# Where the weight sums, the rounding remainders and the token sums of a fused attention and two-MLP kernel are made: one rearrangement across five engines

## The reference

```python
x = attn_out.transpose(0, 2, 1, 3).reshape(B * S, H * D)       # 2304 x 512
x = (sigmoid(x @ w_gate) * (x @ w_val)) @ w_out1               # 512 -> 1536 -> 512
h = x @ w_in                                                   # 512 -> 2048
out = (h * clip(h + 3, 0, 6) / 6) @ w_out2                     # 2048 -> 512
```

## Time and profile before

| | us |
|---|---|
| median of 3 runs | 1125.98 (1125.51 to 1126.51) |
| the profiled execution | 1120.71 |
| its span in the profile | 1118.9 |
| PE busy | 1074.4 (96%) |
| DVE, ACT, POOL busy | 724.5, 619.2, 526.6 |

### The profile page before, as it was taken

How to read it: one execution, slowest core, us unless ns; L and a number is a source line. 1 busy time by engine, 2 the same in 40 slices (tenths; PEclk the granted TensorE clock), 3 DMA queues, 4 the chain that set the end, 5 groups by cost and what they waited for, 6 DMA issues and landing times.

```text
span 1118.9 us, 20482 instructions
## 1 busy us (share of the span) xinstructions
PE 1074.4 (96%) x6784; PEld 995.7 (89%) x6784; DVE 724.5 (65%) x1541; ACT 619.2 (55%) x1376; POOL 526.6 (47%) x521
## 2 busy tenths in 40 slices
PE   5999999999999999999998988899999999999998
PEld 3668999999999999999998987888987889889887
DVE  5986766777776777776647445665558555675553
ACT  5787676677676677667554333533334433453333
POOL 6896666667666667666545656452223000010000
PEclk8999999999999999999999989999999999999999
DMA  8554334334334334333123755465543544454421
GB/s 183 130 129 96 93 93 120 92 93 120 93 93 120 92 92 121 93 93 100 58 66 104 247 198 196 169 226 152 159 128 99 179 116 120 113 161 122 118 61 57
DMA packets 124460, 136.99 MB, mean 122 GB/s; under 512 B 10448, under 2 KB 89808, under 8 KB 123344
## 3 DMA queue, kind: packets, MB, share of 16 engines
q1 hardware_dynamic: 124368, 135.83, 43.2%
HBM read 116.40 MB, written 19.40 MB: 121 GB/s over the span
## 4 chain that ended last, share of the span: by engine, by line
PE 89%; DVE 6%; issue 2%; DMA 1%; ACT 1%; SPq 0%; POOL 0%; DVEq 0%; ACTq 0%
PE ps L726 83%; PE ps L767 4%; PE ps L781 1%; DVE raw L1612 1%; DVE XC L1506 1%; DMA stage<-w_gate 1%; DVE Cb L1608 1%; DVE prob L1419 0%; DVE G_lo L1616 0%; DMA qk_st<-qk_t 0%; DVE AS L1514 0%; DVE AS L1515 0%; DVE AS L1516 0%; DVE Y L1586 0%; DVE h_lo L1429 0%
## 5 line engine op out<-in xcount | busy, mean ns | idle before, releaser
L726 PE MATMUL ps<-x_hi,WG 128*128 128x288 f32 x1536 | 323.7, 297 | 0.8 <-DVE pt_lo L1367 0.3
L726 PEld LDWEIGHTS ps<-x_hi,WG 128*128 128x128 f32 x1536 | 251.2, 188 | 3.1 <-issue 1.2
L726 PE MATMUL ps<-x_lo,WG 128*128 128x288 f32 x768 | 226.1, 294 | 0.0
L726 PE MATMUL ps<-XC,WC 128*128 128x384 f32 x1008 | 206.2, 340 | 10.1 <-ACT Cb L1263 3.8
L726 PEld LDWEIGHTS ps<-XC,WC 128*128 128x128 f32 x1008 | 182.2, 190 | 27.9 <-issue 11.5
L1608 DVE TENSOR_TENSOR Cb<-ps,Cb 128x384 f32<-128x384 f32 x192 | 102.4, 554 | 137.7 <-PE ps L726 94.3
L726 PE MATMUL ps<-h_hi,WO 128*128 128x288 f32 x768 | 170.4, 304 | 13.9 <-DVE h_lo L1429 13.6
L617 POOL TENSOR_TENSOR WG<-stage,WG 128x512 fp32r<-128x512 f32 x96 | 127.6, 1343 | 117.0 <-ACT WG L1088 117.0
L726 PE MATMUL ps<-wo,G_hi 128*128 128x512 f32 x540 | 168.0, 392 | 0.0
L644 POOL TENSOR_SCALAR prob<-prob,rscale 128x128 f32<-128x128 f32 (+4 forms) x160 | 110.9, 711 | 77.6 <-DVE rscale L1379 77.6
L726 PEld LDWEIGHTS ps<-x_lo,WG 128*128 128x128 f32 x768 | 144.2, 188 | 0.5
(11 more groups left out here) (127 smaller groups left out, 1989.2 us busy)
## 6 DMA issues: line engine op xcount, KB each, us to landing
WC<-w_in_parts SPq DMA_DIRECT2D x154, 256.0 KB, 2.7
stage<-w_out SPq DMA_DIRECT2D x64, 256.0 KB, 3.4
qk_st<-qk_t SPq DMA_DIRECT2D x54, 288.0 KB, 4.2
w_in_parts<-WC SPq DMA_DIRECT2D x8, 1792.0 KB, 7.4
stage<-w_gate SPq DMA_DIRECT2D x48, 256.0 KB, 3.3
stage<-w_val SPq DMA_DIRECT2D x48, 256.0 KB, 3.2
qn_st<-q_n SPq DMA_DIRECT2D x16, 256.0 KB, 3.3
raw_in<-w_in SPq DMA_DIRECT2D x16, 256.0 KB, 7.8
```

The lines of the kernel that those rows point to most:

```text
L726: return pe.matmul(o, l, r, start=start, stop=stop, skip_group_check=True)
```

## The change

1. DVE makes the sums of both pairs of a lone quarter in its first half, even e in slot 1 and odd e in slot 2. ACT rounds the odd pair at the start of the second half.
2. POOL makes remainders in seven pieces of 128x256, where it had one of 128x1280 and two of 128x256; the even pair's now come ahead of two weight blocks in the first half, the odd pair's ahead of the four blocks of the second half.
3. SP writes both pairs and loads the next two in the second half: the even pair after its first block, the odd pair after its last.
4. The token sums `XS` get five buffers (two lie where `stage` was). Those of the second chunk are made in one go after the last w_out2 tile is cut, those of the third one for each step. SP loads three w_out2 tiles for each step, and POOL holds the third tile until the seven products of step 0 are done.
5. Products 2 to 6 of step 0 go to banks 0 to 4 and don't wait for a bank; the first output units then wait for all eight additions of step 0.
6. `x_high2` and `x_lower2` come one slot later around a chunk's boundary, and the last two `x_lower2` of the first chunk come behind all copies of O0 to O7.

```diff
+    XS = [sb("XS0", [P, 2, CH], F32)]
...
-    XS = [sb(f"XS{j}", [P, 2, CH], F32) for j in two]
+    XS += [sb(f"XS{k}", [P, 2, CH], F32) for k in (1, 2)]
...
+    top[0] = stage_at
+    XS += [sb(f"XS{k}", [P, 2, CH], F32) for k in (3, 4)]
...
         def prod_bank(s, i):
-            return ps[:, MLP + (PROD * s + i) % 2, 0:CH]
+            return ps[:, MLP + (PROD * s + i) % 2 if s or i < 2 else i - 2, 0:CH]
...
+            def prepared_next(e):
+                write_parts(e)
+                if e + 2 < FP:
+                    load_raw_in(e + 2)
...
                     for x, (ahead, k) in enumerate([x for slot in CUT[p] for x in slot]):
-                        if prep is not None and prep >= 1 and x == 1:
-                            write_parts(prep - 1)
-                            if prep + 1 < FP:
-                                load_raw_in(prep + 1)
+                        if prep is not None and p == 1 and x == 1:
+                            prepared_next(prep - 1)
...
+                if prep is not None and p == 1:
+                    prepared_next(prep)
...
             for s in range(n_steps):
-                for x in (2 * s + NST, 2 * s + NST + 1):
+                for x in range(3 * s + 2 if s else NST, 3 * s + 5):
...
-            def low_ws(r, p, cut):
+            def low_ws(r, p, cut, alone):
                 for i, slot in enumerate(CUT[p]):
+                    if alone and i == (0 if p else 3):
+                        prep_lo(prepared(r, p))
...
             def prep_lo(e):
                 j = e % 2
                 pool.wait_ge(p_hi, 3 * (e + 1))
-                for at, src in ((slice(0, 5), AS[j][:, :, :]), (slice(5, 6), raw_in[j][0][:, 0:2 * P].unsqueeze(1)),
-                                (slice(6, 7), raw_in[j][1][:, 2 * P:4 * P].unsqueeze(1))):
-                    pool.tensor_tensor(WC[j][:, at, 1, :], src, WC[j][:, at, 0, :].bitcast(F32), ALU.subtract).then_inc(p_lo, 1)
+                sources = [AS[j][:, k, :] for k in range(len(SUMS))] + [raw_in[j][0][:, 0:2 * P], raw_in[j][1][:, 2 * P:4 * P]]
+                for k, src in enumerate(sources):
+                    pool.tensor_tensor(WC[j][:, k, 1, :], src, WC[j][:, k, 0, :].bitcast(F32), ALU.subtract).then_inc(p_lo, 1)
...
             for x, f in enumerate(used):
+                if x == 2:
+                    pool.wait_ge(c_prod, PROD)
...
                 for k in range(len(SUMS)):
-                    m = len(SUMS) * (c - 1) + k
-                    if m >= 2:
-                        pool.wait_ge(xs_lo, PROD * ((m - 2) // len(SUMS) + 1) + SUMS[(m - 2) % len(SUMS)] + 1)
+                    if c == 1:
+                        pool.wait_ge(w_done, n + NST)
+                    else:
+                        pool.wait_ge(c_prod, PROD * (FP * (c - 1) + 2 + k))
+                        pool.wait_ge(xs_lo, PROD * c)
                     a, b, op = x_sum_of(k, c)
-                    pool.tensor_tensor(XS[m % 2][:, :, :], a, b, op).then_inc(xs_next, 1)
+                    pool.tensor_tensor(XS[k][:, :, :], a, b, op).then_inc(xs_next, 1)
...
+                if first and c == 0:
+                    pe.wait_ge(c_add, 8)
                 if first and c >= 1:
                     pe.wait_ge(o_left, CT * (c - 1) + t + 1)
...
                 alone = not (scoring or old)
+                if alone and p == 1:
+                    prep_hi(prepared(r, p))
...
-                    if alone and i == 2 - p:
+                    if alone and p == 0 and i == 2:
                         prep_hi(prepared(r, p))
...
                 for i in range(QT):
-                    if alone and i == 1 - p:
-                        e = prepared(r, p)
+                    if alone and p == 0 and i in (1, 2):
+                        e = prepared(r, i - 1)
                         prep_sums(e)
-                        first_sums({0: (0, 1), 2: (2, 3), 4: (4,)}.get(e, ()))
+                        first_sums({0: (0,), 1: (1,), 2: (2,), 3: (3,), 4: (4,)}.get(e, ()))
...
-                            for x in {0: (0, 1, 2), 2: (3,), 4: (4,), 6: (5,), 7: (6,)}.get(j, ()) if not has_next_quarter(r) else ():
+                            for x in {0: (0, 1, 2), 2: (3,), 4: (4,)}.get(j, ()) if not has_next_quarter(r) else ():
                                 x_lower2(0, x)
...
+            x_lower2(0, 5)
+            x_lower2(0, 6)
             for s in range(n_steps):
...
                 if s >= 1:
                     g_low(s - 1, 2)
                     times_relu(s - 1, 3)
+                if ends:
+                    x_lower2(c, 4)
                 added(s, 1, 0, 1, 0)
```

More of the change, by code:

```diff
@@ L77, in attention_and_mlps @@
     Y = sb("Y", [P, DT, B * S], F32)
+    stage_at = top[0]
     stage = [sb(f"stage{j}", [P, BANK], F32) for j in range(NST)]
@@ L163, in attention_and_mlps @@
     raw_in = [[sb(f"raw_in{j}{i}", [P, BANK], F32) for i in two] for j in two]
+    top[0] = stage_at
+    XS += [sb(f"XS{k}", [P, 2, CH], F32) for k in (3, 4)]
+    assert top[0] <= region
     parts = nc.dram_tensor("w_in_parts", (FP, P, PROD * 2 * 2 * P), F32, kind="Internal").ap()
@@ L355, in x_source @@
             k = SUMS.index(i)
-            return XF[:, k, :, :] if c == 0 else XS[(5 * (c - 1) + k) % 2][:, :, :]
+            return XF[:, k, :, :] if c == 0 else XS[k][:, :, :]
         def prod_bank(s, i):
-            return ps[:, MLP + (PROD * s + i) % 2, 0:CH]
+            return ps[:, MLP + (PROD * s + i) % 2 if s or i < 2 else i - 2, 0:CH]
         def out_place(c, t):
@@ L438, in load_raw_in @@
                                  by_row_tile(w_in)[:, :, f * P:(f + 1) * P]).then_inc(p_ld[e % 2], DMA)
+            def prepared_next(e):
+                write_parts(e)
+                if e + 2 < FP:
+                    load_raw_in(e + 2)
             def write_parts(e):
-                sp.wait_ge(p_lo, 3 * (e + 1))
+                sp.wait_ge(p_lo, PROD * (e + 1))
                 sp.dma_start(parts[e, :, :], WC[e % 2][:, :, :, :].rearrange("p a b c -> p (a b c)").bitcast(F32)).then_inc(p_wr[e % 2], DMA)
@@ L528, in _ @@
                 load_out2(x)
-            write_parts(FP - 1)
             def store(c, tiles):
@@ L681, in step @@
                     phi_by_z(n)
-                low_ws(r, p, cut)
-                if not (scoring or old):
-                    prep_lo(prepared(r, p))
+                low_ws(r, p, cut, not (scoring or old))
             wait_qk(0)
@@ L704, in _ @@
             for x, f in enumerate(used):
+                if x == 2:
+                    pool.wait_ge(c_prod, PROD)
                 if x == EARLY:
-                    pool.wait_ge(p_lo, 3 * FP)
+                    pool.wait_ge(p_lo, PROD * FP)
                     pool.wait_ge(xs_lo, PROD)
@@ L981, in product @@
                 if i == 0 and s < 2:
-                    pe.wait_ge(p_lo, 3 * (FP - 1 + s))
+                    pe.wait_ge(p_lo, PROD * (FP - 1 + s))
                 elif i == 0:
@@ L988, in product @@
                     pe.wait_ge(f_y, OU * (n_pairs + 1) - 1 + g)
-                else:
-                    s0, i0 = divmod(g - 2, PROD)
+                elif g >= PROD:
+                    s0, i0 = divmod(g - 2, PROD) if g >= PROD + 2 else (0, (1, 0)[g - PROD])
                     if i0 < 2:
@@ L1303, in _ @@
                     x_high2(c + 1, 0)
-                    x_high2(c + 1, 1)
                 relu(s, 1)
                 if next_x:
-                    x_high2(c + 1, 2)
+                    x_high2(c + 1, 1)
                 g_high(s, 1)
                 if next_x:
-                    x_high2(c + 1, 3)
+                    x_high2(c + 1, 2)
                 if ends:
@@ L1315, in _ @@
                 if next_x:
-                    x_high2(c + 1, 4)
+                    x_high2(c + 1, 3)
                 if ends:
@@ L1322, in _ @@
                     leave(c - 1, 4)
+                if next_x:
+                    x_high2(c + 1, 4)
                 relu(s, 3)
@@ L1511, in prep_sums @@
                 if e >= 2:
-                    dve.wait_ge(p_lo, 3 * (e - 1))
+                    dve.wait_ge(p_lo, PROD * (e - 1))
                 (a11, a12), (a21, a22) = [[t[:, k * 2 * P:(k + 1) * 2 * P] for k in two] for t in raw_in[j]]
@@ L1638, in _ @@
                     x_lower2(c + 1, 0)
-                    x_lower2(c + 1, 1)
                 times_relu(s, 1)
@@ L1644, in _ @@
                 if next_x:
-                    x_lower2(c + 1, 2)
+                    x_lower2(c + 1, 1)
                 added(s, 5, 2, 4, 5)
                 if next_x:
-                    x_lower2(c + 1, 3)
+                    x_lower2(c + 1, 2)
                 times_relu(s, 2)
@@ L1651, in _ @@
                 if next_x:
-                    x_lower2(c + 1, 4)
+                    x_lower2(c + 1, 3)
             g_low(n_steps - 1, 2)
```

## The result

The changed kernel takes 1116.09 us (median of 4 runs, 1114.99 to 1117.08) where the kernel before, run beside it, takes 1125.74 (4 runs, 1123.46 to 1126.51): a ratio of 0.9917, 95% interval 0.9899 to 0.9935, or 9.65 us gained. The forecast was 1114.8. A second timing beside other runs of before gave 1113.89, ratio 0.9911 (0.9895 to 0.9926).

What follows compares the result with a forecast made beforehand. PE was taken as the bound, with 89% of the chain. Terms 5.3 + 1.9 + 5.0 - 1.0 = 11.2 us took the profiled 1120.7 to 1109.5, or 1114.8 against the median; range 1100 to 1121.

Steps and rivals of the forecast that it cites:

- the four terms: Lone quarters 5.3 us gained, second MLP's start 1.9 gained, boundaries 5.0 gained, mid-chunk sums 1.0 lost.
- The three waits for `h_lo` go: Lone quarters: PE's three waits and their low clock vanish, 19.7 us removed.
- V0 waits for the odd sums: Second to fourth lone quarters: late odd raw tiles make PE wait 5.0, 2.1 and 2.6 us.
- the working: Lone-quarter reckoning: even write at 616.0, odd raw tiles usable 17.0 us later, 14.4 us standing in place of 19.7.
- The lone quarters gain 5.3: Lone quarters: 10.0 us of waits and 4.4 of low clock replace 19.7; bounds 16.0 to -0.1.
- The start of the second MLP gains 1.9: Second MLP's start: 14.7 us in place of 16.6, from 1 lost to 4.5 gained.
- DVE's way of 11.3 us: Second MLP's start: DVE's time to all eight additions, 2.8 + 6.5 + 2.0 us, taken as 12.1 beside POOL's cuts.
- Boundaries gain 5.0: Chunk boundaries: 0.2 of each 2.7 us idle stays, 5.0 us gained, bounds 2.7 and 5.4.
- Five sums in mid-chunk lose 1.0: Mid-chunk: five token sums of 2.15 us in a row cost PE 1.0 us, between 0 and 4.
- The rival of 4 us lost: Mid-chunk: five sums in a row block DVE, PE loses 4 us, not 1; time 1117.8, chance 0.11.
- The rival in which the odd raw tiles are hidden anyway: Lone quarters: V0 passes in time, only 0.3 of 19.7 us stays; time 1100.7, chance 0.17.
- The slower rival: Lone quarters: raw tiles later still, nothing gained from 2.3 us delay, 1134.1 at 5; chance 0.05 loss, 0.07 no change.

Runs made afterwards that it cites:

- loads first: Changed kernel, with SP asking for a pair's next raw tiles ahead of that pair's write instead of behind it: 1108.54 us.
- writes last: Changed kernel, with both writes of a lone quarter behind all its loads (raw tiles and w_out1 blocks): 1105.07 us.
- large pieces: Changed kernel, with POOL's remainders in one piece of 128x1280 and two of 128x256 as before: 1112.88 us.
- two banks: Changed kernel, with step 0 of the second MLP in two PSUM banks again, without the wait for all eight additions: 1110.48 us.
- early w_out2: Changed kernel, with SP's first three w_out2 loads ahead of the last write: 1114.18 us.
- after again: Changed kernel without an edit, timed a second time: 1113.89 us, ratio 0.9911.
- Token sums alone: Kernel before, plus only five token-sum buffers, sums in mid-chunk and the later `x_high2` and `x_lower2`: 1116.69 us, ratio 0.9930.
- the two other edits: Changed kernel with both writes behind the loads, plus step 0 in two banks and first w_out2 loads ahead of the last writes: 1102.58 us.

## Why the prediction was right, point by point

The direction and the mechanism in the lone quarters were right, and the time lay 1.3 us from the forecast. The time was partly luck: two of the four terms came out well below their size, and the medians show some 3 us that no term accounts for.

- *The three waits for `h_lo` go.* Right: none is left in after.
- *V0 waits for the odd sums, since the raw tiles stand behind the even write, three blocks and the odd write.* Right, and shown by loads first and writes last. The tiles were usable 18.7, 17.9 and 17.5 us after the even write, where the working had 17.0; the sums took 3.4 to 4.1 us, inside its 2.1 to 4.7. The even write itself came at 619.17, where the working had 616.0; 1.9 of these 3.2 us are the later beginning of the quarters, the rest POOL's way to it. The waits were 2.93, 2.32 and 3.63 us, 8.9, where it had 5.0, 2.1 and 2.6, 9.7. The first lone quarter has no gap (0.3 expected).
- *The lone quarters gain 5.3.* Too much: by the profiles it is 1.9. The step that was mis-sized is the cost of the late queue. The working let only DVE wait behind it, but ACT does too: a w_out1 block behind the even write held a gate copy for 2.39 us. PE, late by that and by the low clock behind it, waited less for V0 there: with large pieces, where the gate copy's gap was 0.35 us, V0's was 4.70, near the 5.0 of the working; with gate-copy gaps of 2.1 to 3.8 us (after, two banks, early w_out2, after again) it was 2.9 to 3.6. Idle time was 11.3 us for 10.0, and the half-speed stretches lost 1.7, 3.1 and 1.7 us, 6.5 for 4.4 (each is its length times what its clock lacks, as from 642.60: 6.20 x 0.50). So 17.8 us stand in place of 19.7, inside the bounds given (16.0 to -0.1).
- *The start of the second MLP gains 1.9.* Wrong in sign: 1.0 lost, at the edge of its bounds. The first gap is 1.1 us (0.4 expected), from the first product to the first output unit 738.90 - 725.10 = 13.8 (12.1), and 2.7 are lost to the clock behind it (2.2): 17.6 in place of 16.6. The step that failed is DVE's way of 11.3 us, for which 0.8 us more were taken beside POOL's cuts: four operations of 0.50 to 0.55 us took 0.96 to 1.45 there, and in early w_out2, with most of the cuts out of the way, the stretch was 12.4 us, near the 12.1. Two banks in step 0 gave 4 and 5 us back, so the five banks together with their wait for all eight additions cost more than they save; the two were not tried apart.
- *Boundaries gain 5.0.* Right: 5.4, all of it.
- *Five sums in mid-chunk lose 1.0.* They lost nothing. One DVE operation did take 2.20 us beside them, as the earlier trace rows suggested, but PE was busy throughout. The rival of 4 us lost fell. By the lock of the Trainium skill (SBUF — State Buffer, section SBUF: two separate sides) each sum can hold a VectorE instruction for its whole length. The trace agrees with that (2.20 us beside a sum of 2.1) and not with the price that the rival gave it.

By the profiles that is 1.9 - 1.0 + 5.4 = 6.3 us of the 7.6 between them from the lone quarters on, where 11.2 were forecast. The profile of before lies 5 us under its median, and by medians 9.65 were gained, some 3.3 more than the terms. Token sums alone gained 7.5 by medians, where the boundaries' term is 5.4, so part of the excess may lie in that part, but 5.4 is inside its interval. Where the 3.3 us come from stays open.

The rival in which the odd raw tiles are hidden anyway (1100.7) fell here, by the queue. With all loads ahead of the writes most of its 25.3 us come: 19.1, and 21.4 with the two other edits, though waits on ACT take the place of DVE's. The slower rival's point, 2.3 us of delay on the queue, was not reached: 0.5 to 1.7 were measured. Its argument had a slip: 22 us for 17 would be rates lower by about a quarter, not a third.

## What to carry to other kernels

On a queue that many engines' data share, ask for what someone waits for before what nobody waits for: moving two large writes behind the loads was worth about as much again as the whole change (19.1 us in place of 9.65). When a transfer is late, list every engine that stands in order behind it; here the forecast saw DVE and missed ACT. A burst through more buffers that ends in one wait for everything can lose to a slower flow through two, as step 0 did here.

## What the runs showed of the hardware that was not expected

- Behind a DMA issue on POOL, a DVE operation on two SBUF inputs can stand still through all of POOL's following back-to-back operations: 7.88 and 8.00 us in one kernel, 7.13 and 8.00 in the other, over nine operations, where its neighbours took 0.45 to 0.64 us. Three of the four began during the issue, the one of 7.13 us 0.55 us after its end. In the first quarter of both kernels the same sequence held it for 2.5 us only, and with the issue behind the run, no `h_lo` in the lone quarters took over 1.6 us. The lock of the Trainium skill (SBUF — State Buffer, section SBUF: two separate sides) holds for one instruction; here it was nine, and why DVE got no turn between them is open.
- A load asked for on SP's queue at 620.94 us was usable at 631.19, while POOL's queue wrote 3.67 MB from 618.2 us: the two queues share the DMA engines, which from 620 to 632 us showed a busy share of 0.85 to 1.15 and moved 214 to 459 GB/s.
- The clock after an idle stretch is not told by its length alone: 0.54 after 2.39 us, 1.00 after 2.32, 0.59 after 3.63.
